# ScalarE's pooled exponentials and VectorE's pooled totals put elsewhere in the attention steps of a fused attention and two-MLP kernel

## What is computed

```python
# q, k, v: (4, 8, 576, 64), factor = 4
q_d, k_d, v_d = mean over groups of 4 positions              # 144 pooled positions
out_d   = softmax(q_d @ k_d.T / 8) @ v_d                       # pooled attention, repeated 4 times
out_local = softmax(q @ k.T / 8 where |i - j| < 4) @ v         # banded local attention
x = out_d.repeat(4) + out_local          -> (2304, 512)
x = ((x @ w1) * (x @ w2)) @ w3 @ w_out                         # first MLP, no nonlinearity but the product
h = x @ w_in;  out = (h * sigmoid(h)) @ w_out2                 # second MLP
```

## Time and profile before

| | us |
|---|---|
| median of 3 runs (lowest, highest) | 818.29 (817.83, 820.70) |
| profiled execution, its own time | 818.61 |
| span of the profiled execution | 816.8 |
| PE busy | 793.5 (97%) |
| DVE busy | 594.7 (73%) |
| ACT busy | 348.2 (43%) |
| POOL busy | 271.8 (33%) |
| mean granted PE clock (share of full) | 0.997 |

### The profile page before, as it was taken

The page is one execution under the profiler, slowest core; times in us unless marked ns, Lnnn a source line. Parts: engine busy times, 40 slices in busy tenths (PEclk is TensorE's granted clock), DMA queues, the critical chain, the costliest instruction groups (busy, mean ns, idle before and its releaser), DMA issues.

```text
span 816.8 us, 13915 instructions
## 1 busy us (share of the span) xinstructions
PE 793.5 (97%) x5400; PEld 716.2 (88%) x5400; DVE 594.7 (73%) x949; ACT 348.2 (43%) x791; POOL 271.8 (33%) x342
## 2 busy tenths in 40 slices
PE   7799999999999999999999999999999999999997
PEld 6678777989998999989999888888889888888986
DVE  6888886677676776886769677679677769757644
ACT  5887867532352223433245233344322344433321
POOL 7887874342214223223313122113113112212100
PEclk9999999999999999999999999999999999999999
DMA  9575643011111111111103131122322112412102
GB/s 322 162 242 199 214 126 124 26 53 53 41 37 53 52 30 49 53 44 35 52 28 129 54 101 52 52 79 94 111 77 79 52 55 78 152 52 85 45 0 78
DMA packets 23041, 69.84 MB, mean 86 GB/s; under 512 B 2496, under 2 KB 2496, under 8 KB 22976
## 3 DMA queue, kind: packets, MB, share of 16 engines
q1 hardware_dynamic: 22832, 68.36, 25.6%
q10 hardware_dynamic: 144, 0.59, 0.2%
HBM read 64.23 MB, written 4.72 MB: 84 GB/s over the span
## 4 chain that ended last, share of the span: by engine, by line
PE 85%; ACT 7%; DVE 4%; issue 2%; DMA 1%; ACTq 0%; DVEq 0%
PE ps L1034 43%; PE ps L1092 25%; PE ps L1063 12%; PE ps L1117 2%; ACT prob_d L492 2%; ACT prob L503 2%; PE ps L1192 1%; ACT pt L439 1%; DVE prob L750 1%; PE ps L1178 1%; DVE low L758 1%; DMA qk<-in_qk 1%; DVE wa L708 1%; ACT w3t L439 0%; DVE totd L782 0%
## 5 line engine op out<-in xcount | busy, mean ns | idle before, releaser
L1034 PE MATMUL ps<-xb,wa 128*128 128x384 f32 x2016 | 405.0, 338 | 0.5 <-DVE mu L862 0.4
L1034 PEld LDWEIGHTS ps<-xb,wa 128*128 128x128 f32 x2016 | 355.0, 188 | 22.6 <-DVE mu L862 1.5
L374 POOL TENSOR_TENSOR rw<-rw 128x256 f32<-128x256 f32 x192 | 166.8, 889 | 451.8 <-DMA rw<-in_sets 338.4
L862 DVE TENSOR_TENSOR mu<-ps,mu 128x384 f32<-128x384 f32 x132 | 73.1, 554 | 120.8 <-PE ps L1034 120.6
L1063 PE MATMUL ps<-g,r 128*128 128x512 f32 (+1 forms) x576 | 124.9, 338 | 2.3 <-issue 2.3
L602 ACT ACTIVATE a<-a 128x384 f32<-128x384 f32 x72 | 37.9, 526 | 188.3 <-DVE a L862 188.3
L1092 PE MATMUL ps<-w2h_even,g 128*128 128x512 f32 x432 | 113.2, 394 | 0.0
L1092 PE MATMUL ps<-w2h_odd,g 128*128 128x512 f32 x432 | 112.5, 393 | 0.0
L708 DVE TENSOR_TENSOR wa<-rw,wa 128x1024 fp32r<-128x1024 f32 x96 | 106.0, 1104 | 4.3 <-ACT wa L439 4.2
L1063 PEld LDWEIGHTS ps<-g,r 128*128 128x128 f32 x576 | 97.7, 188 | 10.9 <-issue 2.9
L1092 PEld LDWEIGHTS ps<-w2h_odd,g 128*128 128x128 f32 x432 | 79.9, 188 | 11.9
(11 more groups left out here) (78 smaller groups left out, 737.7 us busy)
## 6 DMA issues: line engine op xcount, KB each, us to landing
rw<-in_sets SPq DMA_DIRECT2D x48, 512.0 KB, 3.5
w2r<-in_w_out SPq DMA_DIRECT2D x24, 512.0 KB, 3.5
qk<-in_qk SPq DMA_DIRECT2D x15, 576.0 KB, 6.5
vg<-in_vg SPq DMA_DIRECT2D x16, 336.0 KB, 4.2
vw<-in_vw SPq DMA_DIRECT2D x16, 320.0 KB, 3.1
out<-osb SPq DMA_DIRECT2D x18, 256.0 KB, 2.8
wn<-in_w SPq DMA_DIRECT2D x16, 256.0 KB, 4.5
raw<-in_w_out SPq DMA_DIRECT2D x2, 1024.0 KB, 10.0
```

What stands on the lines that cost most here:

```text
L374: nc.gpsimd.tensor_tensor(blocks[:, o, :], blocks[:, a, :], blocks[:, b, :], op).then_inc(done, 1)
L862: nc.vector.tensor_tensor(o, half_bank(k, i), term, ALU.add).then_inc(sum_ready, 1)
L1034: e = nc.tensor.matmul(ps[:, (k + i) % 2, 0:TH], wa[:, k % 2, l, A_SLOT[i], a * P:(a + 1) * P], xb[:, i, r, a, :], start=(i in (0, 1, 4) a ...
```

## The change

In steps s >= 4 ACT makes the pooled exponentials right behind `exps_late`, ahead of `w3_high`, `copy_pt` and `copy_ptd`. In steps 1 to 3 it makes them behind `copy_pt` and `copy_ptd`. On DVE `totals_down` goes ahead of `w3_low` in steps s >= 4; in steps below 4 it goes behind the low halves of w_out (L819). No operation is added or removed, and PE, POOL and SP have the same programs as before.

```diff
@@ ScalarE, step(s)
                 exps_local()
                 exps_late()
+                if s >= FOLD:
+                    exps_down()
                 for q in splits_of(s):
                     w3_high(q)
                 if s > 0:
                     copy_pt()
+                    copy_ptd()
                 if s == 0:
                     act.wait_ge(blank, 2)
-                exps_down()
-                if s > 0:
-                    copy_ptd()
+                if s < FOLD:
+                    exps_down()
@@ VectorE, step(s)
                 if s == 0:
                     min_local(1)
+                if s >= FOLD:
+                    totals_down(s)
                 for q in splits_of(s):
                     w3_low(q)
-                totals_down(s)
                 for n in W_OUT.get(s - 1, ())[0::2]:
                     dve.wait_ge(r3_hi, n + 1)
                     nc.vector.tensor_tensor(r3[:, n, 1, :], raw3[:, n, BANK:], r3[:, n, 0, :].bitcast(F32),
                                             ALU.subtract).then_inc(r3_lo_dve, 1)
+                if s < FOLD:
+                    totals_down(s)
```

## The result

The changed kernel takes 824.09 us in the median of 11 runs (822.18 to 826.65), the kernel before 818.29. That is 5.8 more between the medians; the ratio is 1.0064, with a 95% interval of 1.0053 to 1.0075: slower by 0.64%, against the 3.0 us less that I had forecast and outside of my range. The profiled execution took 825.79, its span is 824.0, 7.2 more than before. In the changed kernel DVE's lines stand two or three higher (L731 is L733, L782 is L784, L702 is L704, L708 is L710, L819 is L822, L750 is L752) and PE's L1178 is L1183.

A forecast was written before the change was run, and what follows sets the result against it. PE, busy 97%, was held in the attention steps only by waits for ACT's ptd; EXTRA steps were an ACT and DVE loop of some 8.5. 3.3 less by step 8, 0.3 more by step 15: 815.3 us, range 812.0 to 818.9.

The forecast's parts named there:

- PE's own pace: Steps 5 to 8: nothing but PE sets the pace, 7.80 us a step, before and after the change.
- 0.1 later: Even late steps on DVE: L731, held behind POOL's L414, lets the EXTRA item start at 127.07 instead of 126.99.
- DVE had got in first wherever both waited: Lock between DVE and POOL: rows 5 and 6 show DVE winning, the ground for taking the middle estimates.
- from P(8) to P(15): Starts of PE's L1178 in steps 8 and 15: the way between them grows by 0.3 us.
- The third rival: Late even steps: POOL's L420 gets ahead of L731, item 1.15 later in six steps; 821.9 us, chance 0.05.
- Totd's exponentials are done at 26.9, ahead of it: Step 2: pooled exponentials end before POOL's L414 starts at about 27.1, so mask starts at about 27.2.
- The gain at P(4): Start of PE's L1178 in step 4: forecast at 42.5, against 45.38 before.
- the second rival: Steps 2 to 4: early gain mostly lost to held totd, POOL's lateness or clock; about 817.4 us, chance 0.23.
- T(4): Start of the first local exponential in step 4: forecast at 36.8 in place of 39.49.
- P(5) = P(4) + 7.80: Step 4 runs at PE's pace: L1178 of step 5 starts at 50.3, 3.3 us earlier than before.
- The clock: PE ahead of step 4's L1178: clock falling in a 1.7 us wait, costing up to 1.4 us.
- That costs nothing: ACT's new order in steps 4 to 15: L1178 stays at T + 5.71, no cost or gain on PE.

The follow-up runs named there:

- The last kernel: Kernel before with the change's steps 1 to 3, POOL's scalings exchanged, EXTRA item and step 4's low half of w_out ahead of totd: 811.30 us, ratio 0.9907.
- The exchange of POOL's scalings with the early half: Kernel before with the change in steps 1 to 3 only, and POOL's L420 ahead of L414 in steps 1 to 15: 813.88 us, ratio 0.9942.
- the early half alone: Kernel before with the change in steps 1 to 3 only, later steps as before: 817.71 us, ratio 0.9988.
- The wait on POOL: Changed kernel with one wait added: POOL's L420 waits, from step 4 on, for the end of L731 of the same step: 817.38 us, ratio 0.9986.
- ACT's part alone: Changed kernel with DVE's totals_down back behind w3_low from step 4 on, ACT's order staying changed: 820.52 us, ratio 1.0020.
- the late half: Kernel before with the change in steps 4 to 15 only, steps 1 to 3 as before: 825.49 us, ratio 1.0072.

## Why the prediction was wrong

- **What bounds the stage** was read rightly in steps with an item: the loop of ACT and DVE. The last kernel, made from that reading, brought ten of eleven steps to 7.80 (the other takes 7.95). But the 7.80 of the others was called PE's own pace, and ACT's new order was said to gain nothing on PE. It gained 0.15 in each of steps 5 to 7: the pace had been set by the way from turn_local over pt and the pooled exponentials to ptd.
- **"0.1 later" for an even step** is the step that failed. I followed L731 through L414's lock (while DVE or POOL runs such an instruction, the other engine's waits to its end) correctly (1.38 measured; the item up at T + 5.94 where I had 5.9 to 6.0) and then took the item's own length, 0.95, for granted; it took 1.90. My ground was that DVE had got in first wherever both waited. The rows for that the earlier trace rows held two kinds: DVE's one instruction waiting for POOL, with nothing behind it that needed the lock, and two of DVE's running on with POOL coming up beside them. None had what the change makes: an instruction of DVE that has waited, with POOL's waiting behind it, and a second of DVE's behind that. There POOL was next. It costs 0.95 in each of four steps and as much in step 4 (1.63 in place of 0.68), where the low half of w_out stands in the item's place; so from P(8) to P(15), where I had 0.3 more, 5.5 more came, the slow clock at 88 included. The third rival had L420 getting in one place too early, ahead of L731 and not of the item, and I gave it 0.05; its price of 1.15 in six steps was near what came.
- **"Totd's exponentials are done at 26.9, ahead of it"** is the other step that failed. They were seen at 27.05, L414 was there at 27.00. With an estimate of 0.2 between two events, each built from a chain of rows, I took the favourable order as the likeliest. In step 3 the margin was not there at all, since the two L819 no longer ran as one: the first had waited for L395, so L399 got in between them (34.56, 0.66), and DVE was done only at 35.8. The gain at P(4) was 0.9 and not 2.9. This is the second rival, to which I gave 0.23. The exchange of POOL's scalings with the early half shows that L414 was what stood between: with it out of the way T(4) is 36.42, though the steps that make it up are off by 0.6 and 0.4 against each other. P(5) = P(4) + 7.80 failed as well: step 4 has the same queue as an even step with an item, and P(4) to P(5) took 9.34.
- **The clock** I had only as a risk ahead of P(4), as a part of the second rival; there it came in the profile of the early half alone, not in the changed kernel's. In the changed kernel's two slow stretches came behind longer waits of PE, at 88 and 142, and made some 3 of the 7.2. The wait on POOL took both away together with the held items. That the gaps bring the slow stretches is argued from their place behind them; which gap has one behind it stays open, since gaps of the same length had full clock behind them.
- **"That costs nothing" for ACT's new order**: ptd and L1178 did stay at T + 5.71. But through w3_high's later end ACT's part costs 0.1 to 0.3 in an even step by itself, as the run with ACT's part alone shows (steps 8, 10, 12 and 14: 9.05, 8.90, 8.80 and 8.86, against 8.92, 8.77, 8.54 and 8.52).

## What to carry to other kernels

When an instruction is moved to where two engines share a lock, follow the queue for one more instruction on each side than the one that is moved: who waits behind the holder, and who comes up behind him. An engine's result that nobody wants soon (here POOL's L414 and L420) should be started late on purpose, by order or by a wait, when its lock stands in the way of the critical chain; one added wait was worth some 6.4 us here. An early finish of something off the path (invd) is not free, for it starts what depends on it. And a steady pace of a busy engine is not yet its own pace: look whether each round has the same small wait in it (here 0.17 for ptd).

## What the runs showed of the hardware

A DVE instruction with two SBUF operands waits for the end of POOL's running one, and POOL's for DVE's; the Trainium skill (SBUF — State Buffer, "Who interferes with whom") says so, and L733 behind L414 (1.38 in place of 0.63) now shows it for the case that no row had shown. Totd, of 72x4 elements and 0.17 alone, was held likewise, for up to 1.25. Who is next was new. Where DVE's first instruction had not waited, its second followed at once and POOL's waited for both: L733 0.66, L704 0.95, L420 2.37 in step 13. Where DVE's first had itself waited for POOL, POOL's next got in between: L733 1.38, L420 1.59, L704 1.90 in step 14; likewise L822, L399, L822 in step 3. L420 was issued before DVE's second instruction both times, so the order of issue alone doesn't decide it. All ten traces agree up to 150 us, wherever two such instructions of DVE follow each other without a gap and POOL's comes up during the first; whether it is the waiting of DVE's first instruction that decides, or that POOL's two came right behind each other, the runs don't separate. The clock's slow stretches differ between executions with the same gaps: behind the gap ahead of P(4) of 1.57 to 1.59 the clock stayed full in the changed kernel's profile and fell to 0.50 in that of its early half; behind that ahead of P(15) it fell to 0.57 in the changed kernel's (2.31) and stayed full in the late half's (2.33). The changed kernel's 11 runs have mean granted clocks from 0.991 (at 826.65 us, the slowest) to 0.998 (at 822.44 and 822.82); in between time and clock go together only loosely.
